# Attention row sums by way of DRAM instead of TensorE transposes and PSUM copies

## The chip, the cores and the metric

The kernel runs on one core of one Trainium2 chip. The metric is the device time of one execution in microseconds (us), lower is better. TensorE is PE in the profile, VectorE is DVE, ScalarE is ACT, GpSimd is POOL and SyncE is SP, which here only issues the DMAs.

## The reference

Everything is float32. Attention runs over 16 heads of 768 tokens with head dimension 64; a query sees only the keys that fall in its hash bucket (6 sign bits of a projection). Two feed-forward blocks follow, over 1536 tokens.

```python
q_bucket = sum((q @ proj > 0) * powers);  k_bucket = sum((k @ proj > 0) * powers)
scores = where(q_bucket == k_bucket, q @ k.T / sqrt(64), -1e9)
attn = exp(scores - max(scores))
attn = attn / (sum(attn) + 1e-9)
x = attn @ v                                   # heads joined: 1536 x 512
x = (s * relu(x @ w_in)**2 + b) @ w_out        # 512 -> 2048 -> 512
out = (((x @ w1) * (x @ w2)) @ w3) @ moe2_w_out
```

## The kernel before, in words

Every float32 product is made of three (or, for the weighted sum, two) matmuls in the fast fp32r format, on a high part and a low part of each operand: ACT writes the high part (a copy), and DVE or POOL the low part (operand minus high part).

The attention stage takes the first 304 us. Its unit of work is a tile of 128 queries against all 768 keys; a head has 6 tiles, and a loop body, `pair`, does two heads, 12 tiles (t = 0 to 11). For a tile: PE makes the scores in PSUM (`scores`, L893 and L899), DVE takes the row maximum (`top_of`, L728) and from it scale and bias (`exp_at_of`, L735), ACT does the exponential into `prob` and, in the same instruction, leaves the 128 row sums in `rsum` (`exps`, L501), PE transposes `prob` in two parts of three blocks (`turn`, L910), ACT copies each part as high part (`pt_high`, L524), DVE subtracts for the low part (`pt_low`, L742). A unit is three tiles, 384 queries, so a head has two units and a pair four (units 0 to 3). PE multiplies a unit by V (`weighted`, L923) in three thirds, one per tile, during the unit after it; the result lies in two halves of the partitions in PSUM, ACT copies one half (`o_copy`, L511), DVE adds the other (`o_add`, L765) into `o_sum`.

Every engine works its own list in program order, and semaphores tie the lists. What is done when is written out by hand in `pair` of each engine (ACT L548, DVE L777, PE L947, POOL L392, SP L257). The engines run ahead of each other: at step t DVE takes the maximum of tile t+3, and ACT does the exponential of tile t+2.

The part that the change touches brings 1/(row sum) to the output. The row sums have the query on the partition, the output has it in the free dimension. Before, at t = 1, 4, 7 and 10 DVE adds epsilon to three row-sum columns (`row_sums`, L748) and takes the reciprocal (`inverse_sums`, L755); at t = 2, 5, 8 and 11 PE transposes each column, broadcast to 128 columns, into the PSUM bank `m_ps` (`inverse_rows`, L932), and ACT copies 64 rows of it to `r_sb` (`r_copy`, L518). POOL multiplies `o_sum` by it into `x_raw` (`x_of`, L367). PE then reuses `m_ps` for the hash projections of the next head (`dots`, t = 0, 1, 6, 7; L881 to L884), which DVE turns to bits (`bit_rows`, L721) and SP copies to `km` (`copy_bits`, L232).

POOL's list in a pair is: `x_of` unit 2 of the pair before, scale the queries of a head to come (`scale_q`, L343), `v_lo` (L358), `x_of` unit 3 of the pair before, `q_lo` and `k_lo` (L348, L353), `x_low` of the pair before (L373), `x_of` unit 0, `v_lo`, `scale_q`, `x_of` unit 1, `q_lo`, `k_lo`. ACT's `x_high` (L531) stands at t = 6 and needs all four units of the pair before; `x_low` needs it. PE's `weighted` needs `v_lo` of its head when it begins the head's first unit (at t = 3 and t = 9).

SP's list in a head is: `copy_bits`, `copy_q_hi` (L226), `load_v` (L220), `load_qk` (two DMAs of 384 KB, after `k_lo`, L216). An instruction of SP that waits holds back all DMAs behind it.

After attention PE multiplies two weight matrices (`fused`, L988), then come the first feed-forward block (to about 600 us) and the second. These are stages of matmuls without gaps.

Of the kernel before, what the change touches and what calls it, by code (L numbers as in the profile page):

```python
# [11 lines left out]
P = 128  # L12
# [29 lines left out]
def attention_mlp(nc, qk, v, proj, w_in, w_out, s, b, w12, w3t, w_out2, out):  # L42
    with ExitStack() as ctx:
# [16 lines left out]
        with ExitStack() as a:  # L60
# [9 lines left out]
            r_sb = sb("r_sb", [P, 2, HALF], F32, a)  # L70
# [12 lines left out]
            rsum = sb("rsum", [P, 2, 3], F32, a)  # L83
            rsum_e = sb("rsum_e", [P, 2, 3], F32, a)
            rinv = sb("rinv", [P, 2, 3], F32, a)
# [50 lines left out]
        m_ps = psum[:, 7, 0:HALF]  # L136

# [31 lines left out]
        rrow_done = sem("rrow_done")  # L169
        r_copied = sem("r_copied")  # L170
# [37 lines left out]
        def _(sp):  # L208
# [48 lines left out]
            def pair(pr, last=False):  # L257
                for k in range(2):
# [12 lines left out]
            with sp.Fori(1, PAIRS - 2) as pr:  # L271
# [3 lines left out]
            for k in range(2):  # L275
# [3 lines left out]
                load_v(h + 2, k)  # L279
                load_w(2 + k, k, w_out2[:, (2 + k) * WCH:(3 + k) * WCH])  # L280
            pair(PAIRS - 1, last=True)
            for k in range(2):
                load_w(W3 + k, k, w3t[k])
# [25 lines left out]
        def _(pool):  # L309
# [51 lines left out]
            def x_of(u, unit):  # L361

                pool.wait_ge(o_sum_done, u + 1)
                pool.wait_ge(r_copied, u + 1)
                rows = slice(0, HD) if unit < 2 else slice(HD, P)
                at = slice((unit % 2) * HALF, (unit % 2 + 1) * HALF)
                pool.tensor_tensor(x_raw[rows, at], o_sum[rows, unit % 2], r_sb[rows, unit % 2],  # L367
# [24 lines left out]
            def pair(pr, first=False, last=False, before_last=False):  # L392

                if not first:
                    x_of(4 * pr - 2, 2)
# [4 lines left out]
                if not first:  # L400
# [6 lines left out]
                    x_of(4 * pr - 1, 3)  # L407
# [12 lines left out]
                x_of(4 * pr, 0)  # L420
# [11 lines left out]
                x_of(4 * pr + 1, 1)  # L432
# [46 lines left out]
        def _(act):  # L479
# [13 lines left out]
            def exps(n, t, u):  # L493
# [4 lines left out]
                if t % 3 == 0:  # L498

                    after(act, rsum_done, u - 1)  # L500
                act.activation(prob[:, t % 3], score[t % 2], ACT.Exp, bias=exp_at[:, t % 2, 1:2],  # L501
                               scale=exp_at[:, t % 2, 0:1],
                               accum_out=rsum[:, (t // 3) % 2, t % 3:t % 3 + 1]).then_inc(exp_done, 1)
# [617 lines left out]
```

## Time and profile before

| | |
|---|---|
| median of 3 runs | 818.06 us (817.85 to 819.87) |
| profiled execution | 818.39 us, its span 816.5 us |
| granted TensorE clock, mean | 1.0 of full speed (2.4 GHz) |
| PE busy | 778.7 us, 95% |
| DVE busy | 481.5 us, 59% |
| ACT busy | 383.7 us, 47% |
| POOL busy | 232.4 us, 28% |
| DMA | 42.17 MB, 14095 packets |

The span is the time from the first to the last record of the profiled execution; 1.9 us of that execution's time lie outside it. Busy shares are means over stages that differ: DVE and ACT are nearly full in attention and idle for more than half of what follows. Durations of an instruction include its start and its tail, so instructions that follow each other on an engine overlap a little in the lists.

### The profile page before, as it was taken

The page shows a single profiled execution, that of the slowest core. Times are in us where ns is not written, and L with a number is a line of the kernel's source. Part 1 is how long each engine was busy: PE and PEld are TensorE (multiplying, and loading weights), DVE is VectorE, ACT ScalarE, POOL GpSimd, SP SyncE. Part 2 cuts the span into 40 slices and gives each one's busy share as a digit, 9 for nine tenths or more (in the row PEclk, how much of TensorE's full clock was granted, in tenths as well). Part 3 has the DMA queues.
Part 4 walks back from the last instruction along what each step waited for, and adds up shares of the span by engine and source line. Part 5 has one row for each costly group of instructions (what it writes and reads, how often), then busy time and mean ns, then how long its engine had stood idle before and what let it go on. Part 6 is the DMA issues. An engine that isn't in the chain of part 4 may idle for free.

```text
span 816.5 us, 11692 instructions
## 1 busy us (share of the span) xinstructions
PE 778.7 (95%) x3776; PEld 632.6 (77%) x3776; DVE 481.5 (59%) x838; ACT 383.7 (47%) x718; POOL 232.4 (28%) x150
## 2 busy tenths in 40 slices
PE   3999999999989879999999999999999999999998
PEld 2787778777777768888888888888887888888886
DVE  4899999999989961156665656656576211210220
ACT  2788889888889963344231232323143211211221
POOL 3345555545565454563220211202022000000000
PEclk9999999999999999999999999999999999999999
DMA  5342223232242122233110101101010000001001
GB/s 147 75 97 62 64 61 80 79 81 63 61 119 71 44 78 65 90 103 104 52 51 1 52 0 51 51 1 51 1 53 0 1 26 26 1 14 39 0 0 51
DMA packets 14095, 42.17 MB, mean 52 GB/s; under 512 B 2386, under 2 KB 4434, under 8 KB 14066
## 3 DMA queue, kind: packets, MB, share of 16 engines
q1 hardware_dynamic: 14066, 41.79, 17.9%
q8 instruction: 17, 0.28, 0.1%
q14 instruction: 12, 0.10, 0.0%
HBM read 34.61 MB, written 3.15 MB: 46 GB/s over the span
## 4 chain that ended last, share of the span: by engine, by line
PE 73%; DVE 11%; issue 7%; ACT 5%; DMA 1%; DVEq 0%; SPq 0%; POOL 0%; ACTq 0%
PE psum L984 53%; PE psum L1071 8%; DVE top L728 4%; PE psum L910 3%; PE psum L923 3%; DVE pt_lo L742 3%; ACT prob L501 2%; PE psum L899 2%; PE psum L893 2%; ACT pt_hi L524 1%; DVE x_lo L846 1%; DVE exp_at L735 1%; DMA stage<-in_w_out 1%; PE psum L884 1%; DVE qm L721 1%
## 5 line engine op out<-in xcount | busy, mean ns | idle before, releaser
L501 ACT ACTIVATE prob<-psum,exp_at 128x768 f32<-128x768 f32 x96 | 96.5, 1005 | 29.8 <-DVE exp_at L735 29.8
L742 DVE TENSOR_TENSOR pt_lo<-psum,pt_hi 128x384 fp32r<-128x384 f32 x192 | 98.1, 552 | 11.1 <-ACT pt_hi L524 9.6
L728 DVE TENSOR_REDUCE top<-psum 128x1 f32<-128x768 f32 x96 | 91.0, 948 | 4.3 <-PE psum L899 4.0
L618 ACT ACTIVATE relu<-psum 128x512 f32<-128x512 f32 x48 | 28.6, 597 | 137.3 <-PE psum L984 137.3
L910 PE MATMUL psum<-ident,prob 128*128 128x128 f32 x576 | 85.1, 281 | 7.3 <-DVE pt_lo L742 6.9
L984 PE MATMUL psum<-x_hi,w_c 128*128 128x512 f32 (+1 forms) x288 | 90.6, 396 | 0.0
L984 PE MATMUL psum<-x_hi,w_b 128*128 128x512 f32 (+1 forms) x288 | 90.6, 396 | 0.0
L524 ACT ACTIVATE pt_hi<-psum 128x384 fp32r<-128x384 f32 x192 | 84.2, 495 | 11.0 <-PE psum L910 10.1
L869 DVE TENSOR_TENSOR ab<-psum,a_sb 128x512 f32<-128x512 f32 x24 | 16.6, 692 | 121.3 <-ACT a_sb L668 121.3
L823 DVE SCALAR_TENSOR_TENSOR relu<-psum,relu 128x512 f32<-128x512 f32 x48 | 33.1, 690 | 87.8 <-ACT relu L618 82.7
L910 PEld LDWEIGHTS psum<-ident,prob 128*128 128x128 f32 x576 | 65.4, 141 | 22.1 <-DVE pt_lo L742 13.2
L379 POOL TENSOR_TENSOR w_b<-stage,w_b 128x1024 fp32r<-128x1024 f32 x18 | 43.7, 2426 | 129.8 <-ACT w_b L535 129.0
L923 PE MATMUL psum<-pt_hi,vs 128*128 128x384 f32 x192 | 69.2, 361 | 10.2 <-DVE o_sum L765 7.3
L840 DVE TENSOR_TENSOR y_acc<-psum,y_acc 128x512 f32<-128x512 f32 x96 | 61.6, 685 | 8.6 <-PE psum L984 8.6
L923 PE MATMUL psum<-pt_lo,vs 128*128 128x384 f32 x192 | 64.9, 338 | 0.0
L984 PEld LDWEIGHTS psum<-x_hi,w_b 128*128 128x128 f32 x288 | 54.1, 188 | 13.0
L984 PEld LDWEIGHTS psum<-x_hi,w_c 128*128 128x128 f32 x288 | 54.1, 188 | 13.0
L984 PE MATMUL psum<-x_hi,w_a 128*128 (+1 forms) x192 | 60.4, 396 | 0.0
L893 PE MATMUL psum<-both_hi 128*128 128x512 f32 x192 | 58.7, 388 | 1.1 <-ACT prob L501 1.1
L984 PE MATMUL psum<-g_hi,w_c 128*128 128x512 f32 x192 | 59.3, 390 | 0.0
L984 PE MATMUL psum<-g_hi,w_b 128*128 128x512 f32 x192 | 59.2, 390 | 0.0
L984 PE MATMUL psum<-x_lo,w_b 128*128 128x512 f32 (+1 forms) x144 | 57.0, 396 | 0.0
(92 smaller groups left out, 1516.7 us busy)
## 6 DMA issues: line engine op xcount, KB each, us to landing
raw<-in_qk SPq DMA_DIRECT2D x30, 384.0 KB, 5.0
stage<-in_w_out SPq DMA_DIRECT2D x12, 512.0 KB, 3.4
stage<-in_w3t SPq DMA_DIRECT2D x8, 512.0 KB, 3.2
stage<-in_w_in SPq DMA_DIRECT2D x8, 512.0 KB, 3.3
stage<-in_w SPq DMA_DIRECT2D x8, 512.0 KB, 3.2
raw_v<-in_v SPq DMA_DIRECT2D x16, 192.0 KB, 2.6
qm<-both_hi SPq DMA_DIRECT2D x16, 192.0 KB, 2.7
out<-out_sb SPq DMA_DIRECT2D x12, 256.0 KB, 2.0
```

The lines of the kernel that those rows point to most:

```text
L379: pool.tensor_tensor(lo, stage[:, slot, :], hi.bitcast(F32), ALU.subtract).then_inc(w_lo_done, 1)
L501: act.activation(prob[:, t % 3], score[t % 2], ACT.Exp, bias=exp_at[:, t % 2, 1:2], scale=exp_at[:, t % 2, 0:1], accum_out=rsum[:, (t // 3 ...
L524: act.activation(pt_hi[:, u % 2, 3 * part:3 * part + 3, (t % 3) * P:(t % 3 + 1) * P], turned[part].rearrange("p (j q) -> p j q", j=3), ACT ...
L728: dve.tensor_reduce(top[:, t % 2, 1:2], score[t % 2], AX.X, ALU.max, negate=True).then_inc(top_done, 1)
L742: dve.tensor_tensor(pt_lo[at], turned[part].rearrange("p (j q) -> p j q", j=3), pt_hi[at].bitcast(F32), ALU.subtract).then_inc(pt_lo_done, 1)
L823: dve.scalar_tensor_tensor(relu2[:, f], psum[:, 2 * (k % 2) + f, :], 0.0, relu[:, f], ALU.max, ALU.mult).then_inc(relu2_done, 1)
L840: dve.tensor_tensor(at, psum[:, 4 + m, :], at, ALU.add).then_inc(y_add_done, 1)
L893: pe.matmul(score[t % 2][:, at], both_hi[:, par, 0, q], both_hi[:, par, 1, at], start=True, stop=False)
L910: tr = pe.transpose(turned[part][:, j * P:(j + 1) * P], prob[:, t % 3, blk * P:(blk + 1) * P], ident[:, :])
L923: mm = pe.matmul(o_ps, vs[:, (unit // 2) % 2, j], part[:, unit % 2, j], start=(j == 0 and part is pt_hi), stop=(j == TILES - 1 and part is ...
L984: mm = pe.matmul(psum[:, bank, :], lhs, rhs, start=(i == 0), stop=(i == len(terms) - 1))
L1071: mm = pe.matmul(psum[:, 4 + k, :], p[:, f, rows], w[:, f], start=(f == 0 and i == 0), stop=(f == FT - 1 and i == 2))
```

## The change

Row sums are collected for a whole head: `rsum`, `rsum_e` and `rinv` get six columns instead of three, and epsilon and reciprocal are done once per head, at t = 4 and t = 10. The transposes by PE and the copies by ACT are gone. In their place SP writes the 128 x 6 reciprocals to a row of a DRAM tensor (`sums_out`, 128 pieces of 24 bytes, one per partition), waits for that, and reads the row of 3072 bytes back into 64 partitions of `r_sb` (`sums_in`). In that row the queries stand as (p j), p the place in a tile and j the tile, so `x_of` reads `r_sb` with a step of six elements. SP's list in a head becomes `copy_bits`, `copy_q_hi`, `load_v`, `sums_out`, `load_qk`, `sums_in`. Waits that went with the old way are replaced: PE's first `dots` of a head waits for the bits of the head before, and DVE's `o_add` may now run three units ahead of `x_of` instead of one. Near the end of attention two weight loads (w3t) move into the last pair on SP. The loops of SP and DVE are partly unrolled.

```diff
-            r_sb = sb("r_sb", [P, 2, HALF], F32, a)
+            r_sb = sb("r_sb", [P, SEQ], F32, a)
...
-            rsum = sb("rsum", [P, 2, 3], F32, a)
-            rsum_e = sb("rsum_e", [P, 2, 3], F32, a)
-            rinv = sb("rinv", [P, 2, 3], F32, a)
+            rsum = sb("rsum", [P, 2, TILES], F32, a)
+            rsum_e = sb("rsum_e", [P, 2, TILES], F32, a)
+            rinv = sb("rinv", [P, 2, TILES], F32, a)
...
+        r_rows = nc.dram_tensor("r_rows", [HEADS, SEQ], F32)
...
+            def sums_out(h, par, pr):
+
+                sp.wait_ge(rinv_done, h + 1)
+                sp.dma_start(r_rows[h].rearrange("(p j) -> p j", j=TILES), rinv[:, par]).then_inc(r_out[par], 16)
+
+            def sums_in(h, par, pr):
+
+                sp.wait_ge(r_out[par], 16 * (pr + 1))
+                after(sp, x_done, 2 * h - 2)
+                sp.dma_start(r_sb[HALVES[par]],
+                             r_rows[h:h + 1].broadcast_to([HD, SEQ])).then_inc(r_in[par], 16)
+
...
                     if not last:
                         copy_q_hi(h + 2, k)
                         load_v(h + 2, k)
+                    if last and k == 1:
+                        load_w(W3 + 1, 1, w3t[1])
+                    sums_out(h, k, pr)
+                    if not last:
                         load_qk(h + 4, k)
+                    elif k == 0:
+                        load_w(W3, 0, w3t[0])
+                    sums_in(h, k, pr)
...
-            with sp.Fori(1, PAIRS - 2) as pr:
+            for pr in range(1, PAIRS - 2):
                 pair(pr)
...
+                sums_out(h, k, PAIRS - 2)
                 load_w(2 + k, k, w_out2[:, (2 + k) * WCH:(3 + k) * WCH])
+                sums_in(h, k, PAIRS - 2)
             pair(PAIRS - 1, last=True)
-            for k in range(2):
-                load_w(W3 + k, k, w3t[k])
...
-            def x_of(u, unit):
+            def x_of(u, unit, pr):
 
                 pool.wait_ge(o_sum_done, u + 1)
-                pool.wait_ge(r_copied, u + 1)
+                pool.wait_ge(r_in[unit // 2], 16 * (pr + 1))
                 rows = slice(0, HD) if unit < 2 else slice(HD, P)
                 at = slice((unit % 2) * HALF, (unit % 2 + 1) * HALF)
-                pool.tensor_tensor(x_raw[rows, at], o_sum[rows, unit % 2], r_sb[rows, unit % 2],
+                third = slice(3 * (unit % 2), 3 * (unit % 2) + 3)
+                pool.tensor_tensor(x_raw[rows, at].rearrange("d (j p) -> d j p", p=P),
+                                   o_sum[rows, unit % 2].rearrange("d (j p) -> d j p", p=P),
+                                   r_sb[rows].rearrange("d (p j) -> d j p", j=TILES)[:, third],
                                    ALU.mult).then_inc(x_done, 1)
...
-                if t % 3 == 0:
-
-                    after(act, rsum_done, u - 1)
+                if t % 6 == 0:
+
+                    after(act, rsum_done, h - 1)
                 act.activation(prob[:, t % 3], score[t % 2], ACT.Exp, bias=exp_at[:, t % 2, 1:2],
                                scale=exp_at[:, t % 2, 0:1],
-                               accum_out=rsum[:, (t // 3) % 2, t % 3:t % 3 + 1]).then_inc(exp_done, 1)
+                               accum_out=rsum[:, (t // 6) % 2, t % 6:t % 6 + 1]).then_inc(exp_done, 1)
...
-            def r_copy(u, unit):
-
-                act.wait_ge(rrow_done, u + 1)
-                after(act, x_done, u - 3)
-                rows = slice(0, HD) if unit < 2 else slice(HD, P)
-                act.activation(r_sb[rows, unit % 2], m_ps[rows], ACT.Copy).then_inc(r_copied, 1)
...
-                    if t % 3 == 2:
-                        r_copy(4 * pr + t // 3, t // 3)
...
-            def inverse_sums(u, unit):
-                dve.wait_ge(rsum_done, u + 1)
-
-                after(dve, rrow_done, u - 1)
-                dve.reciprocal(rinv[:, unit % 2, :], rsum_e[:, unit % 2, :]).then_inc(rinv_done, 1)
+            def inverse_sums(h, par, pr):
+                dve.wait_ge(rsum_done, h + 1)
+
+                after(dve, r_out[par], 16 * pr)
+                dve.reciprocal(rinv[:, par, :], rsum_e[:, par, :]).then_inc(rinv_done, 1)
...
-                after(dve, x_done, u - 1)
+                after(dve, x_done, u - 3)
...
-                    if t % 3 == 1:
-                        row_sums(n + 1, u, t // 3)
+                    if t % 6 == 4:
+                        row_sums(n + 1, h, k)
                     if ahead:
                         exp_at_of(n + 3, t + 3)
-                    if t % 3 == 1:
-                        inverse_sums(u, t // 3)
+                    if t % 6 == 4:
+                        inverse_sums(h, k, pr)
 
             pair(0, first=True)
-            with dve.Fori(1, PAIRS - 1) as pr:
+            pair(1)
+            with dve.Fori(2, PAIRS - 1) as pr:
                 pair(pr)
...
-            def inverse_rows(u, unit):
-
-                pe.wait_ge(rinv_done, u + 1)
-                for j in range(3):
-                    tr = pe.transpose(m_ps[:, j * P:(j + 1) * P],
-                                      rinv[:, unit % 2, j:j + 1].broadcast_to([P, P]), ident[:, :])
-                tr.then_inc(rrow_done, 1)
...
-                            after(pe, r_copied, 2 * h)
+                            pe.wait_ge(bits_done, 2 * h + 2)
...
-                        if t % 6 == 2 and not (last and k == 1):
-                            pe.wait_ge(bits_done, 2 * h + 4)
-                        else:
-                            pe.wait_ge(r_copied, u)
-                        inverse_rows(u, t // 3)
```

## Rows read from the trace of the kernel before

**Rows 1.** Engines' busy us, two stretches (PE, PEld, DVE, ACT, POOL, PEclk, DMA, GB/s).
```profile
165.00:210.00 45.00, 42.95 (x259) 35.51 (x260) 42.00 (x86) 39.60 (x83) 23.50 (x17) 1.00 0.26 63
...
400.00:600.00 200.00, 200.00 (x869) 162.85 (x869) 120.61 (x180) 55.40 (x85) 28.80 (x12) 1.00 0.09 29
```

**Rows 2.** Groups by line in one pair, 165.1 to 199.5 us (busy, mean ns | idle before).
```profile
L501 ACT ACTIVATE prob<-psum,exp_at 128x768 f32<-128x768 f32 x12 | 12.1, 1008 | 2.9 <-DVE exp_at L735 2.9
...
L735 DVE SCALAR_TENSOR_TENSOR exp_at<-top 128x2 f32<-128x2 f32 x12 | 3.4, 280 | 0.3
...
L932 PE MATMUL psum<-ident,rinv 128*128 128x128 f32 x12 | 2.0, 276 | 0.1
...
L518 ACT ACTIVATE r_sb<-psum 64x384 f32<-64x384 f32 x4 | 2.0, 489 | 0.3 <-PE psum L932 0.2
```

**Rows 3.** Timeline, DVE at t = 0 and t = 1 (start, duration).
```profile
164.20 0.69 DVE L721 TENSOR_SCALAR qm<-psum,bit_from,bit_weight 64x384 fp32r<-64x384 f32 x1
...
165.11 1.02 DVE L742 TENSOR_TENSOR pt_lo<-psum,pt_hi 128x384 fp32r<-128x384 f32 x2
...
167.03 0.69 DVE L721 TENSOR_SCALAR qm<-psum,bit_from,bit_weight 64x384 fp32r<-64x384 f32 x1
...
168.27 1.02 DVE L742 TENSOR_TENSOR pt_lo<-psum,pt_hi 128x384 fp32r<-128x384 f32 x2
```

**Rows 4.** Timeline, the end of t = 2 and the start of t = 3.
```profile
169.51 0.49 ACT L518 ACTIVATE r_sb<-psum 64x384 f32<-64x384 f32 x1 [0.22 <-PE psum L932]
...
170.02 0.48 ACT L511 ACTIVATE o_part<-psum 64x384 f32<-64x384 f32 x1
...
170.62 0.56 DVE L765 TENSOR_TENSOR o_sum<-psum,o_part 64x384 f32<-64x384 f32 x1 [0.27 <-ACT o_part L511]
...
171.46 0.44 PE L923 MATMUL psum<-pt_hi,vs 128*128 128x384 f32 x1 [0.70 <-DVE o_sum L765]
```

**Rows 5.** Timeline, t = 6: `x_high`, `x_low` and DVE's `exp_at`.
```profile
179.91 0.85 ACT L531 ACTIVATE x_hi<-x_raw 128x768 f32 x1
...
181.11 1.83 POOL L373 TENSOR_TENSOR x_lo<-x_raw,x_hi 128x768 f32 x1 [3.63 <-ACT x_hi L531]
...
181.34 1.62 DVE L735 SCALAR_TENSOR_TENSOR exp_at<-top 128x2 f32<-128x2 f32 x1
```

**Rows 6.** Timeline, from the reciprocals at t = 10 to the next pair's t = 3.
```profile
193.21 0.18 DVE L755 RECIPROCAL rinv<-rsum_e 128x3 f32<-128x3 f32 x1
...
195.31 1.15 SPq L216 DMA_DIRECT2D raw<-in_qk  x2
...
196.72 1.02 POOL L367 TENSOR_TENSOR x_raw<-o_sum,r_sb 64x384 f32<-64x384 f32 x1 [1.64 <-DVE o_sum L765]
...
201.15 1.47 POOL L343 TENSOR_TENSOR raw<-raw,scale_col 128x768 f32<-128x768 f32 x1 [3.41 <-DMA raw<-in_qk]
...
202.78 1.01 POOL L358 TENSOR_TENSOR vs<-raw_v,vs 128x384 fp32r<-128x384 f32 x1 [0.16 <-POOL raw L343]
...
205.86 0.44 PE L923 MATMUL psum<-pt_hi,vs 128*128 128x384 f32 x1 [0.64 <-DVE o_sum L765]
```

**Rows 7.** DMA issues by line (count, KB each, median us to landing).
```profile
stage<-in_w_out SPq DMA_DIRECT2D x12, 512.0 KB, 3.4
...
qm<-both_hi SPq DMA_DIRECT2D x16, 192.0 KB, 2.7
out<-out_sb SPq DMA_DIRECT2D x12, 256.0 KB, 2.0
```

**Rows 8.** Chain that ended last, 0 to 370 us (start, us): two DMAs.
```profile
2.09 3.13 DMA pj<-in_proj
...
231.08 5.70 DMA stage<-in_w_out
```

**Rows 9.** Timeline, the end of attention.
```profile
307.27 1.83 POOL L373 TENSOR_TENSOR x_lo<-x_raw,x_hi 128x768 fp32r<-128x768 f32 x1 [1.02 <-ACT x_hi L531]
309.60 0.60 ACT L595 ACTIVATE wc_hi<-psum 128x512 f32 x1 [2.48 <-PE psum L984]
```

More of the change, by code:

```diff
@@ L168, in attention_mlp @@
         rinv_done = sem("rinv_done")
-        rrow_done = sem("rrow_done")
-        r_copied = sem("r_copied")
+        r_out = [sem("r_out0"), sem("r_out1")]
+        r_in = [sem("r_in0"), sem("r_in1")]
         o_part_done = sem("o_part_done")
@@ L394, in pair @@
                 if not first:
-                    x_of(4 * pr - 2, 2)
+                    x_of(4 * pr - 2, 2, pr - 1)
                     pool.wait_ge(x_done, 4 * pr - 1)
@@ L406, in pair @@
                         w_out2_low(2)
-                    x_of(4 * pr - 1, 3)
+                    x_of(4 * pr - 1, 3, pr - 1)
                     pool.wait_ge(x_done, 4 * pr)
@@ L419, in pair @@
                     pool.wait_ge(x_lo_done, pr)
-                x_of(4 * pr, 0)
+                x_of(4 * pr, 0, pr)
                 pool.wait_ge(x_done, 4 * pr + 1)
@@ L431, in pair @@
                     pool.wait_ge(q_scaled, 2 * pr + 5)
-                x_of(4 * pr + 1, 1)
+                x_of(4 * pr + 1, 1, pr)
                 pool.wait_ge(x_done, 4 * pr + 2)
@@ L448, in _ @@
             pool.wait_ge(w_lo_done, W3 + 2)
-            x_of(2 * HEADS - 2, 2)
+            x_of(2 * HEADS - 2, 2, PAIRS - 1)
             pool.wait_ge(x_done, 2 * HEADS - 1)
-            x_of(2 * HEADS - 1, 3)
+            x_of(2 * HEADS - 1, 3, PAIRS - 1)
             pool.wait_ge(x_done, 2 * HEADS)
@@ L491, in v_high, with exps @@
                 act.activation(vs[:, par, :, 0:HD], raw_v[:, par], ACT.Copy).then_inc(v_hi_done, 1)
-            def exps(n, t, u):
+            def exps(n, t, h):
                 act.wait_ge(exp_at_done, n + 1)
                 after(act, turn_done, 2 * n - 4)
-                if t % 3 == 0:
-                    after(act, rsum_done, u - 1)
+                if t % 6 == 0:
+                    after(act, rsum_done, h - 1)
                 act.activation(prob[:, t % 3], score[t % 2], ACT.Exp, bias=exp_at[:, t % 2, 1:2],
                                scale=exp_at[:, t % 2, 0:1],
-                               accum_out=rsum[:, (t // 3) % 2, t % 3:t % 3 + 1]).then_inc(exp_done, 1)
+                               accum_out=rsum[:, (t // 6) % 2, t % 6:t % 6 + 1]).then_inc(exp_done, 1)
             def o_copy(u, unit):
@@ L559, in pair @@
                     if not (last and t > 9):
-                        exps(n + 2, (t + 2) % 12, 4 * pr + (t + 2) // 3)
-                    if t % 3 == 2:
-                        r_copy(4 * pr + t // 3, t // 3)
+                        exps(n + 2, (t + 2) % 12, 2 * pr + (t + 2) // 6)
                     if t % 6 in (3, 4) and not last:
@@ L743, in pt_low, with row_sums @@
                                   pt_hi[at].bitcast(F32), ALU.subtract).then_inc(pt_lo_done, 1)
-            def row_sums(n, u, unit):
+            def row_sums(n, h, par):
                 dve.wait_ge(exp_done, n + 1)
-                dve.tensor_scalar(rsum_e[:, unit % 2, :], rsum[:, unit % 2, :], EPS, None,
+                dve.tensor_scalar(rsum_e[:, par, :], rsum[:, par, :], EPS, None,
                                   ALU.add).then_inc(rsum_done, 1)
-            def inverse_sums(u, unit):
-                dve.wait_ge(rsum_done, u + 1)
-                after(dve, rrow_done, u - 1)
-                dve.reciprocal(rinv[:, unit % 2, :], rsum_e[:, unit % 2, :]).then_inc(rinv_done, 1)
+            def inverse_sums(h, par, pr):
+                dve.wait_ge(rsum_done, h + 1)
+                after(dve, r_out[par], 16 * pr)
+                dve.reciprocal(rinv[:, par, :], rsum_e[:, par, :]).then_inc(rinv_done, 1)
             def rows_of(unit):
@@ L965, in pair @@
                         weighted(u - 1, t // 3 + 3, t % 3, 2 * pr + (t // 3 - 1) // 2)
-                    if t % 3 == 2:
-                        if t % 6 == 2 and not (last and k == 1):
-                            pe.wait_ge(bits_done, 2 * h + 4)
-                        else:
-                            pe.wait_ge(r_copied, u)
-                        inverse_rows(u, t // 3)
             pair(0, first=True)
```

## The prediction

> **What bounds the kernel now.** I first read the busy times by stretch. From 400 to 600 us PE is busy for 200.00 of 200 us at full clock [rows 1]: the feed-forward stages take what PE takes, the change has nothing there, and only a shift of their start can come through. In attention no engine is full by itself: of 45 us from 165 us on, DVE is busy 42.0, PE 42.95, ACT 39.6, POOL 23.5 [rows 1]. So the second view is one pair, which repeats every 34.4 us (`weighted` at t = 3 starts at 171.46 and again at 205.86 [rows 4, 6]). Its groups show a small wait of ACT for DVE's `exp_at` (2.9 us in the pair), and that this tiny instruction has a mean of 280 ns [rows 2]. The timeline explains the mean: at t = 6 one `exp_at` takes 1.62 us, 181.34 to 182.96, and ends when POOL's `x_low` (181.11, 1.83 us) ends [rows 5]. Neither reads PSUM. Read as: a DVE instruction that works on SBUF alone is held up by a running POOL instruction. The chain through a pair goes over all three busy engines in turn: PE and ACT up to the `o_copy` of t = 3, ACT and DVE to t = 6, then the held `exp_at`, DVE to t = 8, PE from t = 9 to t = 12. A microsecond taken from one engine is therefore worth something only in its own part.
>
> **What goes, part by part.** In a pair four groups of transposes (12 x 276 ns as records, which overlap), four ACT copies (4 x 489 ns) and two of four pairs of small DVE instructions go [rows 2]. The two kinds that stay, at t = 4 and 10, work on six columns instead of three: priced at nothing.
>
> (a) DVE at t = 1. At t = 0, without row sums, the time from the end of `bit_rows` (164.20 + 0.69 = 164.89) to `pt_low` (165.11) is 0.22 us; at t = 1, with them, it is 168.27 - 167.72 = 0.55 us [rows 3]. That is 0.33 us. At t = 7 I take 0.25, since part of such a gap is waiting for POOL.
>
> (b) ACT at t = 2 and t = 5. The copy to `r_sb` starts 169.51 after 0.22 us of waiting for PE, and `o_copy` (170.02) is held behind it for 0.51; DVE's `o_add` (170.62) waited 0.27 for that, PE's `weighted` (171.46) 0.70 for `o_add` [rows 4]. Without the copies ACT is earlier by 2 x 0.51 + 0.22 = 1.2 us at t = 6. DVE by itself gains only 0.33 + 0.27 = 0.60 and a few tenths of waiting. But the wait that ends last at t = 6 is for `x_low`, which follows ACT's `x_high` (179.91) [rows 5]. So there ACT's 1.2 counts, with (a)'s 0.33 inside it.
>
> (c) PE at t = 11 gives its three transposes back. A record of 276 ns [rows 2] overlaps the next, so three cost between 0.28 and 0.83 us; I take 0.33, near the low end, as for pipelined matmuls the spacing counts and not the record. At t = 2, 5 and 8 PE waits for DVE afterwards anyway: nothing.
>
> Gross per pair: 1.2 + 0.25 + 0.33 = 1.8 us (both ends: 0.6 us, DVE's two alone; 2.2 us, all four ACT copies at 0.51 and a bit). Over eight pairs 14.4 us.
>
> **What comes.** Two DMAs per head on SP. `sums_out` writes 128 pieces of 24 bytes. Nearest rows: `pj`, also 24-byte pieces, DRAM to SBUF, 3.13 us [rows 8]; a write to DRAM, `out`, 2.0 us [rows 7]. I take 2.5. `sums_in` puts 192 KB into 64 partitions, as `qm` does in 2.7 us [rows 7]. But between the two stands `load_qk`. The reciprocals are there at 193.39, `load_qk` issues from 195.31 to 196.46, so `sums_in` issues at about 196.5, 3.1 us after the reciprocals; the queries and keys are in at 201.15 [rows 6]. How a DMA fares behind them the weights show: alone 3.4 us, issued at 231.08 behind a `load_qk` 5.70 [rows 7, 8]. So `sums_in` takes 2.7 to 5.7 us, and the whole way 5.8 to 8.8 us; I take 7.3.
>
> The Trainium skill (DMA: Bandwidth & Descriptors, "Queues, rings and completion order") says that a DMA's semaphore increment lands only after every earlier write from that DMA engine. The 5.70 us beside 3.4 agree. By that rule alone `sums_in` would land near the upper end, 8.8 us after the reciprocals, and the sum below would lose 1.3 us more in seven pairs, 819 in place of 810; that is inside rival 3.
>
> Who waits: POOL's `x_of` of unit 2, now at 196.72, and behind it in program order `scale_q` (201.15, 1.47 us), `v_lo` (202.78, 1.01 us), then PE's `weighted` at 205.86 [rows 6]. From landing to the end of `v_lo` it is 1.02 + 1.47 + 1.01 + 0.3 between them = 3.8 us. PE will want it about 1.1 us earlier than now (0.33 from (c), 0.33 from (a) and 0.4 from (b) lie between), at 204.75. So a landing by 200.95, 7.5 us after the reciprocals, costs PE nothing; at 7.3 it just fits, at 8.8 it costs 1.3 us per pair. Unit 0 (reciprocals at t = 4) has more room, because `x_low` and its wait for ACT stand ahead of it on POOL. That POOL now works nearer to DVE's small instructions is the price I can't hide: `x_of` of units 0 and 2 starts when a DMA lands and no longer right after an `o_add`, and `exp_at` can meet it. Below nothing if the pattern moves along as it is and `x_low` misses `exp_at` (a gain of up to 1.4); above, one more stall of 1.8 us, the length of `x_low`. I take 0.8 per pair, about one half-covered POOL instruction and a bit.
>
> `x_of` reads its reciprocals with a step of 24 bytes. No row shows POOL with a step. Bounds: 1.0 us as now; 1.83 us, `x_low` with twice the elements [rows 5, 6]. I take 1.0, the row of the same size, and the upper end goes into the slow case.
>
> By the Trainium skill (GPSIMD Engine Reference, "Performance pitfalls for Q7 kernels") a read with a step above 8 bytes costs about half as much again per element, which would make an `x_of` 1.5 us, an estimate from the page, and the slack before `v_lo` 0.5 us smaller: with landings at 7.3 us the sum would be about 2 us higher, 812. No row here shows it.
>
> SP: 2 more issues per head, and its waits for `r_out` end before anything else is due. The semaphore waits of DVE and ACT on sums of two heads ago have long been met.
>
> **The end of attention.** At the last t = 10 the reciprocals no longer hold up PE and `o_copy`; from (b) and (c) I take another 0.8 us. Against it, `x_low` of the last pair now ends 309.10, and ACT's first `wc_hi` (309.60) waits for PE, ending at the same time [rows 9]; about 0.3 us of lateness may come through there. Net 0.5.
>
> **Sum.** Per pair 1.8 - 0.8 = 1.0 us, eight pairs 8.0, and 0.5: 8.5 us off the profiled execution's 818.4 (span 816.5 and 1.9 around it), 809.9. The median of the runs is 0.3 lower than that execution: 809.6, say 810.
>
> **Rivals.**
> 1. Nothing is lost on the way: 14.4 + 0.5, so 803. For: POOL is only half busy [rows 1]. Against: the DMA way just fits.
> 2. The gain is eaten by stalls, 817 to 819: one more `exp_at` under a POOL instruction each pair, 1.8 us against 1.8.
> 3. Slower: the DMA way decides. `x_of` of unit 2 waits for `sums_in`, which lands behind `load_qk`, and pushes `v_lo` behind PE's `weighted` at t = 3. At 8.8 us this costs 1.3 per pair, an `x_of` at 1.83 adds 0.8, and POOL's longer unbroken run one stall of 1.0: 3.1 against 1.8, 1.3 us x 7 = 9 us lost less the 0.5 of the end, so 826 to 827. It turns from gain to loss where landing is more than 7.5 + 1.8 = 9.3 us after the reciprocals, or 8.5 with the longer `x_of`. A part of it, 3 to 6 us slower, is likelier. For: the 5.70. Against: it needs two of three terms at their end.
> 4. The pieces don't go as I read them (a 24-byte write to DRAM far slower than 3.1 us), so that SP itself falls behind with `load_qk`'s successors: 825 and more.
>
> **Chances.** Forecast (804 to 815.6) 0.50, rival 1 0.12, rival 2 0.14, rival 3 0.20, rival 4 0.04. About 0.3% (2.5 us) is what a measurement of this kernel tells from none. So faster 0.62, same 0.14, slower 0.24. The likeliest case's own range is 804 to 815; the range for 8 in 10 goes to 803 below and into rival 3, 821, above.
>
> **What would show it.** In the changed kernel's trace: a pair's period near 33.4 us (34.4 now); `o_add` at t = 3 without a wait for ACT; `sums_in` landing about 7.3 us after the second reciprocal; `x_of` of unit 2 waiting on that DMA and `weighted` at t = 3 still waiting on `o_add` and not on `v_lo`; `x_of` near 1.0 us; the mean of `exp_at` in a pair not above 280 ns by more than 70 (0.8 us over 12). It would be wrong if `weighted` waits for `v_lo`, if `exp_at` grows by 150 ns in its mean (1.8 us per pair), or if the transposes and copies taken away had been hidden even at t = 2 to 6.

## The result, and the profile after

The changed kernel takes 829.69 us (median of 6 runs, 823.86 to 830.43) against 818.21 us for the kernel before in the same job (6 runs, 816.32 to 820.34). The ratio is 1.0118, with a 95% interval of 1.0082 to 1.0155. It is slower by about 1.2%. The forecast was 810, range 803 to 821: sign and range were both wrong. The profiled execution took 830.12 us, its span 828.3.

The loss lies in attention. The first matmul behind it (L984) starts at 314.38 us, where it started at 303.82 before: 10.6 of the 11.8 us by which the span grew. A pair, measured from one `x_low` to the next, takes 37.2 us (187.51 to 224.73) in place of 34.4. The windows of the changed kernel (columns as in [rows 1]) show PE, ACT and POOL less busy than in [rows 1], and the feed-forward stretch as it was. From 175 to 185 us the granted clock is below full speed.

```profile
165.00:210.00 45.00, 41.00 (x229) 33.02 (x227) 42.63 (x74) 34.79 (x73) 19.99 (x15) 0.96 0.36 86
175.00:180.00 5.00, 3.72 (x18) 3.27 (x16) 4.87 (x7) 3.45 (x7) 3.91 (x4) 0.73 0.12 26
180.00:185.00 5.00, 5.00 (x33) 4.62 (x32) 4.64 (x12) 4.84 (x11) 2.14 (x2) 0.93 0.21 53
400.00:600.00 200.00, 200.00 (x869) 162.91 (x868) 122.20 (x180) 53.12 (x83) 28.01 (x12) 1.00 0.09 32
```

DVE alone is as busy as before, although half of its row-sum instructions are gone. The groups of one pair, 187.5 to 224.7 us, say why; they answer to [rows 2].

```profile
L524 ACT ACTIVATE prob<-psum,exp_at 128x768 f32<-128x768 f32 x12 | 11.9, 994 | 6.1 <-DVE exp_at L749 6.1
L749 DVE SCALAR_TENSOR_TENSOR exp_at<-top 128x2 f32<-128x2 f32 x12 | 8.1, 672 | 0.3
L388 POOL TENSOR_TENSOR x_raw<-o_sum,r_sb 64x384 f32<-64x384 f32 x4 | 4.9, 1216 | 9.8 <-DMA r_sb<-r_rows 8.5 <-POOL vs L378 0.7 <-DVE o_sum L779 0.6
L938 PEld LDWEIGHTS psum<-pt_hi,vs 128*128 128x128 f32 x24 | 4.5, 187 | 3.3 <-POOL vs L378 1.6 <-issue 1.3 <-DVE pt_lo L756 0.2
```

`exp_at` costs 8.1 us in the pair where it cost 3.4, and ACT's wait for it went from 2.9 to 6.1. That is +4.7 us. The forecast's own 1.8 of work taken away leaves +2.9 us, and the period grew by 2.8. That the two are so near is in part chance, as the experiments show. The timeline of the changed kernel (selected rows: start, duration, and in brackets the idle time and what ended it) shows where the 4.7 come from, and the way of the reciprocals.

```profile
163.79 0.34 SPq L238 DMA_DIRECT2D r_rows<-rinv  x1
165.63 1.13 SPq L217 DMA_DIRECT2D raw<-in_qk  x2
166.86 0.54 SPq L244 DMA_DIRECT2D r_sb<-r_rows  x1
...
172.32 1.23 POOL L388 TENSOR_TENSOR x_raw<-o_sum,r_sb 64x384 f32<-64x384 f32 x1 [6.76 <-DMA r_sb<-r_rows]
172.63 0.93 DVE L749 SCALAR_TENSOR_TENSOR exp_at<-top 128x2 f32<-128x2 f32 x1
173.71 1.47 POOL L363 TENSOR_TENSOR raw<-raw,scale_col 128x768 f32<-128x768 f32 x1 [0.17 <-POOL x_raw L388]
175.34 1.00 POOL L378 TENSOR_TENSOR vs<-raw_v,vs 128x384 fp32r<-128x384 f32 x1 [0.16 <-POOL raw L363]
175.52 0.85 DVE L749 SCALAR_TENSOR_TENSOR exp_at<-top 128x2 f32<-128x2 f32 x1
176.40 0.56 DVE L779 TENSOR_TENSOR o_sum<-psum,o_part 64x384 f32<-64x384 f32 x1
177.09 1.23 POOL L388 TENSOR_TENSOR x_raw<-o_sum,r_sb 64x384 f32<-64x384 f32 x1 [0.74 <-POOL vs L378]
177.19 0.25 PEld L938 LDWEIGHTS psum<-pt_hi,vs 128*128 128x128 f32 x1 [1.59 <-POOL vs L378]
177.19 0.64 PE L938 MATMUL psum<-pt_hi,vs 128*128 128x384 f32 x1 [1.28 <-DVE o_sum L779]
177.95 0.52 PE L938 MATMUL psum<-pt_hi,vs 128*128 128x384 f32 x1
178.27 0.52 PE L938 MATMUL psum<-pt_lo,vs 128*128 128x384 f32 x1
178.50 1.81 POOL L368 TENSOR_TENSOR both_hi<-raw,both_hi 64x768 fp32r<-64x768 f32 x1 [0.18 <-POOL x_raw L388]
178.91 1.41 DVE L749 SCALAR_TENSOR_TENSOR exp_at<-top 128x2 f32<-128x2 f32 x1
...
187.51 1.83 POOL L396 TENSOR_TENSOR x_lo<-x_raw,x_hi 128x768 f32 x1 [3.28 <-ACT x_hi L547]
187.92 1.44 DVE L749 SCALAR_TENSOR_TENSOR exp_at<-top 128x2 f32<-128x2 f32 x1
```

Each `exp_at` longer than 0.16 us ends with the POOL instruction beside it: 172.63 + 0.93 with `x_of`, 175.52 + 0.85 with the `v_lo` whose end is 176.34, 178.91 + 1.41 with `q_lo`, 187.92 + 1.44 with `x_low`. Before, there was one such meeting of full length, at `x_low` [rows 5]; at t = 3 `exp_at` began at 173.14, 0.05 us ahead of `q_lo`, and was not held; at t = 9 it began 0.21 us ahead. In the kernel before, both places:

```profile
173.14 0.16 DVE L735 SCALAR_TENSOR_TENSOR exp_at<-top 128x2 f32<-128x2 f32 x1
173.19 1.84 POOL L348 TENSOR_TENSOR both_hi<-raw,both_hi 64x768 fp32r<-64x768 f32 x1 [0.85 <-ACT both_hi L486]
...
190.57 0.16 DVE L735 SCALAR_TENSOR_TENSOR exp_at<-top 128x2 f32<-128x2 f32 x1
190.78 1.83 POOL L348 TENSOR_TENSOR both_hi<-raw,both_hi 64x768 fp32r<-64x768 f32 x1 [1.02 <-ACT both_hi L486]
```

The first rows of the changed kernel's timeline are the other half of it. `sums_in` issues at 166.86, behind `load_qk`; `x_of` of unit 2 starts at 172.32, some 8.6 us after the reciprocals were there (163.77), and from there POOL works with gaps of under 0.2 us until 176.34. PE's `weighted` starts at 177.19. Its weight load's wait of 1.59 us is put down to `v_lo`, but `v_lo` was over at 176.34, 0.85 us earlier; what ended last is `o_add` (176.40 + 0.56 = 176.96), which stood on DVE behind the `exp_at` that `v_lo` had held until 176.37. So the late rows reach PE here by way of the held `exp_at`. It is the same at 139.90 and 214.41; at 67.22 and 104.00 `v_lo` itself ended last, 0.05 us before PE. Behind the pause at 177.19 the matmuls have records of 0.52 us and a spacing of 0.32, where they have 0.34 and 0.17 at full clock: the granted clock was at 1.2 GHz for a part of 175 to 180 (mean 0.73). Three stretches of attention show a lower granted clock (65 to 75, 175 to 185 and 250 to 260 us). Behind the pauses of 1.3 us at 104.00, 139.90 and 214.41 it stayed full.

Waits of the changed kernel from 0 to 380 us (who, for what: us in all, times, the longest) and its DMA issues:

```profile
POOL x_raw L388 <- DMA r_sb<-r_rows: 64.0, 14, 7.5
ACT prob L524 <- DVE exp_at L749: 37.8, 42, 6.1
PE psum L938 <- DVE o_sum L779: 8.3, 6, 2.4
PEld psum L938 <- POOL vs L378: 8.3, 5, 1.9
```

```profile
r_sb<-r_rows SPq DMA_DIRECT2D x16, 192.0 KB, 5.4
r_rows<-rinv SPq DMA_DIRECT2D x16, 3.0 KB, 1.4
```

Two causes are thus possible for the held `exp_at`: the late landing, which bunches POOL's work, or the work taken from PE and ACT, which changes who starts when. The experiments separate them. All were timed in three rounds beside the kernel before; every ratio is to that.

### The profile page after: what moved, and what is told of

The parts are those of the page before. It is cut to its first block, busy times and chain, and to the rows that moved or that the text cites. A ratio compares the mean times of both kernels' runs of the same rounds, so it can differ in the third digit from the quotient of the medians.

```text
span 828.3 us, 11229 instructions
## 1 busy us (share of the span) xinstructions
PE 776.8 (94%) x3680; PEld 628.4 (76%) x3680; DVE 492.2 (59%) x806; ACT 372.7 (45%) x686; POOL 238.6 (29%) x150
## 4 chain that ended last, share of the span: by engine, by line
PE 66%; DVE 17%; issue 7%; ACT 4%; DMA 3%; POOL 1%; SPq 1%; DVEq 1%; ACTq 0%; POOLq 0%
PE psum L984 51%; PE psum L1071 8%; DVE top L742 6%; DVE pt_lo L756 6%; DVE exp_at L749 2%; PE psum L925 2%; PE psum L938 2%; ACT prob L524 2%; ACT pt_hi L540 1%; PE psum L914 1%; DVE x_lo L861 1%; PE psum L908 1%; DVE o_sum L779 1%; DMA stage<-in_w_out 1%; DMA raw<-in_qk 1%
## 5 line engine op out<-in xcount | busy, mean ns | idle before, releaser
L925 PE MATMUL psum<-ident,prob 128*128 128x128 f32 x576 | 88.8, 287 | 16.0 <-DVE pt_lo L756 15.3
L925 PEld LDWEIGHTS psum<-ident,prob 128*128 128x128 f32 x576 | 67.3, 144 | 36.3 <-DVE pt_lo L756 26.5
L984 PE MATMUL psum<-x_hi,w_c 128*128 128x512 f32 (+1 forms) x288 | 90.6, 396 | 0.0
L984 PE MATMUL psum<-x_hi,w_b 128*128 128x512 f32 (+1 forms) x288 | 90.6, 396 | 0.0
L884 DVE TENSOR_TENSOR ab<-psum,a_sb 128x512 f32<-128x512 f32 x24 | 16.6, 692 | 121.3 <-ACT a_sb L682 121.3
L984 PEld LDWEIGHTS psum<-x_hi,w_c 128*128 128x128 f32 x288 | 54.1, 188 | 13.0
L984 PEld LDWEIGHTS psum<-x_hi,w_b 128*128 128x128 f32 x288 | 54.1, 188 | 13.0
L984 PE MATMUL psum<-x_hi,w_a 128*128 (+1 forms) x192 | 60.4, 396 | 0.0
L388 POOL TENSOR_TENSOR x_raw<-o_sum,r_sb 64x384 f32<-64x384 f32 x32 | 38.8, 1213 | 71.5 <-DMA r_sb<-r_rows 64.0
L984 PE MATMUL psum<-g_hi,w_c 128*128 128x512 f32 x192 | 59.3, 390 | 0.0
L984 PE MATMUL psum<-g_hi,w_b 128*128 128x512 f32 x192 | 59.3, 390 | 0.0
```

What stands on the lines that cost most here:

```text
L388: pool.tensor_tensor(x_raw[rows, at].rearrange("d (j p) -> d j p", p=P), o_sum[rows, unit % 2].rearrange("d (j p) -> d j p", p=P), r_sb[ro ...
L925: tr = pe.transpose(turned[part][:, j * P:(j + 1) * P], prob[:, t % 3, blk * P:(blk + 1) * P], ident[:, :])
L984: mm = pe.matmul(psum[:, bank, :], lhs, rhs, start=(i == 0), stop=(i == len(terms) - 1))
```

## The experiments

**Without the DMA way.** The changed kernel, with nothing between the reciprocals and `x_of`. `x_of` multiplies by the identity tile, so this kernel leaves out the division:

```diff
 def sums_out / sums_in:  -   (both DMAs)            +   pass
-pool.wait_ge(r_in[unit // 2], 16 * (pr + 1))
-    r_sb[rows].rearrange("d (p j) -> d j p", j=TILES)[:, third],
+    ident[rows].unsqueeze(1).broadcast_to([HD, 3, P]),
```

> The changed kernel without its two DMAs and without the wait of x_of for them; x_of multiplies by a constant tile (the identity), so the division is left out. Theory A (the late landing of the sums holds POOL, whose operations then run unbroken and stall exp_at): the work taken from PE, ACT and DVE is worth its 1.8 us per pair, a pair's period falls to about 32.8 us and the time to 803 to 806. Theory B (the landing is not to blame; with ACT unloaded, POOL's operations that follow ACT start before exp_at in place of behind it, and stall it): period 35 us or more, exp_at still above 450 ns in the mean, time 815 to 828.

Measured 819.40 us, ratio 0.9993 (0.9972 to 1.0013). With all of the removed work gone and nothing in its place, the kernel isn't faster than before. `exp_at` has a total of 46.3 us over attention (31.7 before, 51.7 in the changed kernel), 14.6 more, where by the forecast's sum 14.9 of work were taken away. So the gain is eaten before any DMA comes in. Its timeline at t = 9 of a pair shows a meeting that before did not take place:

```profile
192.01 1.82 POOL L364 TENSOR_TENSOR both_hi<-raw,both_hi 64x768 fp32r<-64x768 f32 x1 [0.61 <-ACT both_hi L504]
192.13 1.72 DVE L744 SCALAR_TENSOR_TENSOR exp_at<-top 128x2 f32<-128x2 f32 x1
```

`q_lo` waits for ACT, and ACT is now ahead: `q_lo` starts 0.12 us in front of `exp_at`, where at t = 9 of the kernel before it came 0.21 us behind it. At t = 3 the order is turned round too (`q_lo` 173.99, `exp_at` 174.26, 1.57 us long).

**DMAs issued, read by no one.** As above (no division either), with both DMAs in their place and no engine waiting for them before the end of attention.

```diff
 sums_out, sums_in as in the changed kernel
+after(sp, r_in[par], 16 * pr)
-pool.wait_ge(r_in[unit // 2], 16 * (pr + 1))
```

> As e1 but with both DMAs issued as in the changed kernel; nobody on POOL waits for them or reads them (division left out). It prices the DMA traffic and SP's waits alone. Theory A: as e1, plus 0 to 1 us. Theory B: as e1 too. A third theory C, that the traffic or SP falling behind is the price: 820 or more where e1 is 803 to 806.

Measured 820.71, ratio 1.0009 (0.9995 to 1.0022). Against the first experiment the traffic and SP's issues cost about 1.3 us, within the intervals. What is left up to the changed kernel, 1.0118 against 1.0009, some 9 us, comes from waiting for the rows and reading them.

**Reading without a step.** The changed kernel, with `x_of` reading `r_sb` in memory order (so the queries get each other's row sums).

```diff
-r_sb[rows].rearrange("d (p j) -> d j p", j=TILES)[:, third],
+r_sb[rows].rearrange("d (j p) -> d j p", p=P)[:, third],
```

> The changed kernel with x_of reading r_sb without a step (the values come out in the wrong order of queries). Prices the 24-byte step: an x_of of 1.21 us should fall to 1.01 us. Theory A: 1 to 3 us less than the changed kernel, 827 to 829, since POOL's unbroken run gets 0.2 us shorter per x_of. Theory B: the same within 1 us of the changed kernel.

Measured 828.42, ratio 1.0109 (1.0078 to 1.0140). `x_of` takes 1.01 us, as before, in place of 1.21; the kernel is faster than the changed one by 0.7 us by the ratios (1.3 by medians of different jobs), inside the intervals. The step is not the loss.

**`sums_in` ahead of `load_qk`.**

```diff
 sums_out(h, k, pr)
+sums_in(h, k, pr)
 load_qk(h + 4, k)
-sums_in(h, k, pr)
```

> The changed kernel with sums_in issued before load_qk in SP's list, so that it does not land behind it. The way from the reciprocals to the landing should fall from 8.6 us to about 5. Theory A: x_of of unit 2 starts 3.5 us earlier, PE's weighted no longer waits for v_lo, and the time falls by half or more of the loss, to 815 to 822. Theory B: 828 to 832, nothing gained.

Measured 828.52, ratio 1.0097 (1.0060 to 1.0134). The landing was brought forward as meant, and it gained 1 to 2 us, inside the intervals. The timeline of this kernel, SP and POOL:

```profile
164.83 0.46 SPq L244 DMA_DIRECT2D r_sb<-r_rows  x1
165.39 1.19 SPq L217 DMA_DIRECT2D raw<-in_qk  x2
...
168.35 1.20 POOL L388 TENSOR_TENSOR x_raw<-o_sum,r_sb 64x384 f32<-64x384 f32 x1 [3.18 <-DMA r_sb<-r_rows]
172.01 1.47 POOL L363 TENSOR_TENSOR raw<-raw,scale_col 128x768 f32<-128x768 f32 x1 [2.46 <-DMA raw<-in_qk]
```

The landing is 3.5 us after its issue, not 5.4, and `x_of` runs at 168.35, out of the way. But `scale_q` then waits for the queries and keys, and `exp_at` is held by that (1.25 us), by both `q_lo` (1.58 and 1.72) and by `x_low` (1.45): its total is 50.3 us, against 51.7. PE has no wait for `v_lo` any more, and no pause of over 0.7 us at `weighted` before 290 us. A stall that was removed was for the most part replaced by another.

**Only ACT's copies away.** The kernel before, transposes kept, division left out. PE's waits for the copies go with them.

```diff
-pool.wait_ge(r_copied, u + 1)           +pool.wait_ge(rrow_done, u + 1)
-if t % 3 == 2:
-    r_copy(4 * pr + t // 3, t // 3)
```

> The kernel before with only ACT's four copies per pair taken away; transposes and row sums stay, x_of multiplies by a constant tile (the division is left out). Theory B (ACT, unloaded, lets POOL's q_lo start ahead of exp_at at t = 3 and t = 9 and stall it for 1.6 us each): exp_at's mean rises from 330 to 450 ns or more and the time is 818 or above, although 15 us of ACT work are gone. Rival D (the stalls of e1 come from DVE's or PE's part of the change): exp_at's mean stays at 330 ns and the time falls to 808 to 812.

Measured 821.58, ratio 1.0023 (0.9999 to 1.0047). Taking 32 ACT instructions of 0.49 us from the kernel before makes nothing faster. `exp_at` goes from 31.7 to 42.3 us in all.

**No DMA way, but ACT's copies back.** The first experiment with 32 copies of the old size, which nobody reads.

```diff
+if t % 3 == 2:
+    spare_copy(t // 3)     # ACT copy, 64 x 384, ident -> r_sb
```

> e1 (no DMAs, division left out) with a spare ACT copy of the same size put back at the place of each copy taken away. Theory B: q_lo again starts behind exp_at, exp_at's mean falls from 482 back to 330 ns; PE's and DVE's share of the gain shows, so the time is below e1's 819.4, at 810 to 815, though ACT has 15 us more to do. Rival D: slower than e1, 822 to 828.

Measured 814.76, ratio 0.9948 (0.9926 to 0.9970). Adding useless work made the first experiment's kernel 4.6 us faster. The group of `exp_at` in the first experiment, then in this one:

```profile
L744 DVE SCALAR_TENSOR_TENSOR exp_at<-top 128x2 f32<-128x2 f32 x96 | 46.3, 482 | 2.7
```

```profile
L751 DVE SCALAR_TENSOR_TENSOR exp_at<-top 128x2 f32<-128x2 f32 x96 | 31.2, 326 | 2.7
```

With ACT's phase put back, `exp_at` is back at the mean of the kernel before (330). By the ratios the gain is 3.7 us, and the two intervals only just part. Where ACT stands relative to DVE decides how often POOL and `exp_at` meet.

**One meeting taken away from the kernel before.** POOL starts `x_low` only after the `exp_at` that it used to hold.

```diff
+pool.wait_ge(exp_at_done, 12 * pr + 10)
 x_low(pr - 1)
```

> The kernel before with one added wait: POOL's x_low starts only when DVE's exp_at of t = 6 is done. Nothing else is changed. If a POOL operation in progress is what holds exp_at, the one stall of 1.46 us per pair goes and x_low ends about 0.4 us later; 7 pairs, 10 us at most, and I expect 808 to 812. If exp_at is long for another reason, 817 to 821.

Measured 822.25, ratio 1.0015 (0.9990 to 1.0040), where 808 to 812 was expected. The stall at t = 6 is gone, and in its place stands one at t = 9, somewhat longer, and in every second pair one more at t = 3 (139.24 and 210.46, 1.8 us each):

```profile
192.06 1.83 POOL L348 TENSOR_TENSOR both_hi<-raw,both_hi 64x768 fp32r<-64x768 f32 x1 [0.70 <-ACT both_hi L487]
192.09 1.81 DVE L736 SCALAR_TENSOR_TENSOR exp_at<-top 128x2 f32<-128x2 f32 x1
```

By the moved phase the engines fall into the next meeting. So I kept POOL from all three places at once: the wait above, and the same wait ahead of both `q_lo`.

```diff
+pool.wait_ge(exp_at_done, 12 * pr + 7)
 q_lo(2 * pr + 2, 0)
...
+pool.wait_ge(exp_at_done, 12 * pr + 10)
 x_low(pr - 1)
...
+pool.wait_ge(exp_at_done, 12 * pr + 13)
 q_lo(2 * pr + 3, 1)
```

**The three waits in the kernel without a DMA way.**

> e1 (no DMAs, division left out) with waits added on POOL: q_lo at t = 3 and t = 9 and x_low at t = 6 start only when the exp_at of that step is done. Theory B: the three stalls of 1.4 to 1.6 us per pair go, exp_at's mean falls under 250 ns, and what was forecast for the work taken away shows at last: 800 to 808. Rival D: about e1's 819.

Measured 800.17, ratio 0.9763 (0.9722 to 0.9804): 19 us faster than the same kernel without the waits. The mean of `exp_at` fell to 277 ns, not below the 250 expected; `scale_q` and others without a wait still hold it.

**The three waits in the kernel before, in the changed kernel, and in the one with `sums_in` first.**

> The kernel before with waits added on POOL: q_lo at t = 3 and t = 9 and x_low at t = 6 start only behind the exp_at of that step. In e7, with x_low's wait alone, the stall of t = 6 went but q_lo's two came (1.8 us at t = 9). Theory B (stalls move to whichever POOL operation then starts just ahead of exp_at): with all three gated exp_at's mean is under 270 ns and the time 806 to 812. Rival E (the kernel before cannot gain from fewer stalls, as e7 says): 818 to 823.

> The changed kernel with the same three waits on POOL. If the stalls on q_lo and x_low were all, it would come to e8's 800 and a few us. But x_of of unit 2 still waits for its DMA, 8.6 us behind the reciprocals, with scale_q and v_lo behind it: those stalls (1.0 and 0.85 us) and PE's wait for v_lo at t = 3 stay, worth 1 to 2 us per pair. So 808 to 816.

> e4 (sums_in issued ahead of load_qk) with the same three waits on POOL; a complete kernel. If the lateness of the sums is what still costs e10, this is 3 to 6 us faster than e10, 803 to 812. If what counts is that load_qk itself is later (scale_q waits for it), it is no faster than e10.

Measured 809.16, ratio 0.9869 (0.9829 to 0.9910), for the kernel before; 814.47, 0.9939 (0.9914 to 0.9963), for the changed one; 810.29, 0.9879 (0.9837 to 0.9921), with `sums_in` first. `exp_at` in the kernel before with the three waits:

```profile
L738 DVE SCALAR_TENSOR_TENSOR exp_at<-top 128x2 f32<-128x2 f32 x96 | 20.0, 209 | 2.2
```

With the waits the difference between the changed kernel and the one before falls from 11.5 us to 5.3. The changed kernel's `exp_at` has a mean of 361 ns there: it is still held by `x_of`, `scale_q` and `v_lo`, which have no such wait. PE still pauses at t = 3 for 1.1 to 1.5 us, behind `v_lo` or what `v_lo` held.

**`exp_at` that can't be held.** The waits give POOL delays of their own. The cleaner test is to change what `exp_at` reads: the row maximum goes to two free columns of PSUM, so that only one of its two inputs is in SBUF. Left out is the zeroing of queries that match no key. The edit also changes the operation from a comparison and a product to two products, so the place of the input is not the only thing that differs.

```diff
-top = sb("top", [P, 2, 2], F32, a)
+ones = sb("ones", [P, 2], F32, a)
+top = [psum[:, 2 * k + 1, 260:262] for k in range(2)]
...
-dve.scalar_tensor_tensor(exp_at[:, t % 2], top[:, t % 2, 1:2].broadcast_to([P, 2]), NO_MATCH,
-                         top[:, t % 2], ALU.is_lt, ALU.mult)
+dve.scalar_tensor_tensor(exp_at[:, t % 2], top[t % 2], 1.0, ones[:, :], ALU.mult, ALU.mult)
```

It was done to the changed kernel, to the kernel before, to the one without a DMA way and to the one with `sums_in` first.

> The changed kernel with the row maximum kept in PSUM and exp_at reading it there beside a constant in SBUF, so that it has one input in SBUF in place of two; the zeroing for queries without any matching key is left out. If POOL holds exp_at by way of exp_at's two inputs in SBUF, no exp_at is over 0.3 us any more whatever POOL does, and the time falls by most of the 36 us of stalls that are on the path: 800 to 812. If exp_at is held for another reason (its output, or its place behind the reduce), 826 to 832.

> The kernel before with exp_at reading the row maximum from PSUM, as e12 (the zeroing for queries without a matching key is left out). exp_at loses 16.6 us of stalls; rsum_e, which reads SBUF, keeps its own. If the stalls were on the path: 804 to 809, near e9. The work taken away by the change is then seen as e13 minus e14.

> e1 (no DMAs, division left out) with exp_at reading PSUM, as e12. Theory: all stalls gone and all work taken away, 795 to 800; against e13 the gain of the work alone, 1 us or more per pair.

> e12 with sums_in ahead of load_qk in SP's list. If the late landing costs by itself (PE's wait for v_lo, 7 to 9 us in e12), this is 2 to 6 us below e12, 797 to 801. If not, 802 to 805.

| top in PSUM, `exp_at` never held | us | ratio (95%) | a pair | the same kernel with top in SBUF |
|---|---|---|---|---|
| kernel before | 808.61 | 0.9870 (0.9822 to 0.9918) | 33.2 | 818.2 |
| changed kernel | 803.21 | 0.9795 (0.9755 to 0.9834) | 33.0 | 829.7 |
| `sums_in` first | 793.86 | 0.9679 (0.9641 to 0.9718) | 31.5 | 828.5 |
| no DMA way | 791.96 | 0.9659 (0.9620 to 0.9698) | 31.5 | 819.4 |

The instruction itself, in the changed kernel with top in PSUM (least, median and greatest duration in ns, over all 96):

```profile
L752 DVE SCALAR_TENSOR_TENSOR exp_at<-psum,ones x96: 147/159/161, 19.0 to 277.9; 128x2 f32<-128x2 f32 x96
```

Not one is longer than 161 ns, although 43 of the 96 start while a POOL instruction runs. The last two kernels came out 3 us below the lower ends that were expected. And the order of the kernels turns over: the same change that costs 11.5 us with an `exp_at` that can be held gains 5.4 without (808.61 to 803.21; the runs don't overlap, the intervals of the two ratios just do), and 14.8 with `sums_in` first. What still parts the changed kernel from the one with `sums_in` first, 9.3 us by the medians, is seen in the first one's waits:

```profile
POOL x_raw L389 <- DMA r_sb<-r_rows: 63.7, 14, 7.7
...
PEld psum L941 <- POOL vs L379: 9.0, 5, 2.2
PE psum L941 <- POOL vs L379: 7.4, 5, 1.8
```

Here `v_lo` does end last, 0.05 us before PE's `weighted`, in all five places.

With `sums_in` first PE waits 1.0 us in all for `v_lo`.

## Why the prediction was wrong

**Right: what the removed work is worth.** The forecast took 1.8 us per pair and 0.5 at the end, 14.9 in all. Where nothing can hold `exp_at`, the kernel before and the one without a DMA way differ by 16.6 us (the extremes of the runs by 12.9 to 20.9), and by 14.8 with the DMAs, read early. A pair goes from 33.2 to 31.5.

**The step that failed** is the price of "that POOL now works nearer to DVE's small instructions": "I take 0.8 per pair", with "one more stall of 1.8" as its upper bound. `exp_at` grew by 4.7 us per pair (8.1 against 3.4). What of this was on the path, the table shows: with `exp_at` never held a pair of the changed kernel falls from 37.2 to 33.0, one of the kernel before only from 34.4 to 33.2. The change thus brought 3.0 us of holding per pair, where 0.8 was taken.

A second term failed beside it, the one set to nothing: "a landing by 200.95, 7.5 us after the reciprocals, costs PE nothing; at 7.3 it just fits". Where nothing is held, the late rows cost 33.0 - 31.5 = 1.5 us per pair. Together, 34.4 - 1.7 for the removed work + 3.0 + 1.5 = 37.2, as measured; the forecast said 33.4. The split takes the two as if they added, and they don't quite: with holding, the early landing gained a pair only 0.6 us or so.

Two things were wrong in the price of the holding.

First, the mechanism was tied to the DMA. I looked for meetings where `x_of` starts on a landing. But `q_lo` and `x_low` are released by ACT, and I had just put ACT 1.2 us earlier without asking what POOL starts with it. In the trace of before, `q_lo` begins at 173.19, directly behind an `exp_at` begun at 173.14. The edit turns that order round. The kernel without a DMA way shows it by itself: 14.6 us of stalls against 14.9 of gain. Only ACT's copies away gives 10.6 us of stalls (31.7 to 42.3) and no gain, and ACT's copies back removes them.

Second, a stall was priced as an addition, of which one more would be the worst. It is a matter of phase: with one meeting taken away the next takes its place, at the same length. With all of them taken away the four kernels of the table gain 10 to 35 us.

**Off in its size: the DMA way.** It took 8.6 us from the reciprocals to `x_of`, inside the bounds of 5.8 to 8.8 and above the 7.3 taken. The write in 24-byte pieces was faster than forecast (1.4 us to landing against 2.5), the read slower (5.4 against 4.2), for the reason given: it was issued behind 768 KB of queries and keys, and in front of them it takes 3.5. The Trainium skill's rule (DMA: Bandwidth & Descriptors, "Queues, rings and completion order"), which the forecast weighed beside its sum, gave 8.8 us for the way; 8.6 is nearer to that than to 7.3. Beyond 7.5 us PE was to wait for `v_lo`. It pauses in five places at t = 3, in two of them for `v_lo` itself and in three for the `o_add` behind the `exp_at` that `v_lo` held. This is near to rival 3's mechanism, and in the kernels without holding it is worth 9.3 us. Of rival 3's three terms, the landing was there, the longer `x_of` only by 0.2 us in place of 0.8, and its stall of 1.0 was too small, like mine. Its time of 826 is 4 us below the result, with the terms in other proportions. In the changed kernel the late rows cost some 9 us too, from 1.0009 to 1.0118. How much of these is stalls, how much PE's pauses and how much the lower clock behind them is not settled: the kernel with `sums_in` first has no such pauses and one drop of the clock (245 to 260 us) in place of three, yet it has stalls nearly as large and is only 1 to 2 us faster.

**The read with a step.** `x_of` went from 1.01 to 1.21 us, one fifth more, with one of its two inputs at a step of 24 bytes. Half as much again, which the forecast weighed from the Trainium skill (GPSIMD Engine Reference, "Performance pitfalls for Q7 kernels"), is too much for this instruction.

**The holding itself** was read rightly from one 1.62 us instruction [rows 5], in its direction: DVE waits for POOL. What was missing is what `exp_at` needs to be free of it: with one of its two inputs in PSUM it is never held. The Trainium skill states this in SBUF — State Buffer, "SBUF: two separate sides": a DVE instruction with two SBUF inputs and a GpSimd instruction that reads SBUF exclude each other for the whole length of the one that began first. The trace agrees (178.91 + 1.41 is the end of `q_lo`), and so does the greatest duration of 161 ns with one input in PSUM. It shows one direction only: POOL held by the 0.16 us of an `exp_at` is not seen (`q_lo` at 173.19 begins 0.05 us into one and takes 1.84 us). Weighed against this change, that rule would have asked of each POOL start on which side of `exp_at` it falls.

**Versions that beat both kernels.** Complete ones are the kernel before with the three waits, 809.16 us, and the changed kernel with `sums_in` first and the three waits, 810.29. Their intervals overlap. The fastest time, 791.96, belongs to a kernel that leaves out the division and the zeroing; with the division in it is 793.86.

## What to carry to other kernels

When an edit makes an engine earlier, list what that engine releases on the others, and look up in the trace what stands within a microsecond of each start. A tiny instruction whose mean is twice its median (330 against 161 ns here) is a sign of something that holds it; first make it unholdable (one input from PSUM, or a wait on the big instruction), since until then every other edit is measured through the change of phase that it brings. A DMA on which a tight chain waits belongs ahead of the bulk loads of its queue, but this shows in the time only once the other stall is gone.

## What the runs showed of the hardware

- A DVE instruction of 128 x 2 with two inputs in SBUF takes 0.15 to 0.16 us alone. Started behind a POOL instruction that reads SBUF it lasts until that one ends, at most 2.33 us in the changed kernel and 2.36 us in the kernel before without ACT's copies. With one of the inputs in PSUM it took at most 0.161 us in 96.
- Two inputs are not the whole condition. The instruction that adds epsilon to the row sums has one input in SBUF and a median of 169 ns in the kernel before, and it was held too: in 10 of 32 it took 0.28 to 1.21 us, as at 202.15, where its 0.50 us end with `scale_q` [rows 6]. The reciprocal, one input as well, was never held in the changed kernel (190 to 193 ns), where only two of 16 started under a running POOL instruction; in the kernel before with top in PSUM eight did, and took 0.16 to 0.17 us. Why these two differ wasn't tested.
- In the changed kernel the pause of 1.3 us before 177.19 was followed by a granted clock of 1.2 GHz: 0.73 as the mean of the 5 us with the pause, 0.93 in the next 5, 1.00 before it. So were the pause of 1.6 us before 67.22 and the one of 2.4 us before 254.50, which itself came 4 us after one of 2.1 us. The pauses of 1.3 us before 104.00, 139.90 and 214.41 were not (1.00 in the 5 us with each and in the next 5), nor one of 1.8 us in the kernel before (301.65). The length of a single pause doesn't tell them apart.
- A write of 128 pieces of 24 bytes to DRAM landed 1.4 us after its issue, less than the 2.0 us of a 256 KB write [rows 7].
